# Filter products of a frequency-domain convolution as pairs of 64-row tiles, two steps at a time

## The chip, the core and the metric

The kernel runs on one core of one Trainium2 chip. The metric is the device time of one execution in microseconds (us), the median of several runs. TensorE, here PE, multiplies a stationary operand, which a weight load (PEld) puts into its array, by a moving operand that streams past it, and writes to PSUM, which has eight banks of 512 fp32 columns. VectorE is DVE, ScalarE is ACT, GpSimd is POOL, and SP is the engine whose queue issues most of the DMA transfers.

## The reference

```python
# x, v: (1, 12480, 128); pos_emb: (12480, 64); w1: (64, 64); w2: (64, 128)
h_mlp = np.maximum(pos_emb @ w1, 0.0) @ w2
h_filt = h_mlp * np.exp(-0.01 * pos)[:, None]
u = x * v
L = 2 * S
Uf = np.fft.rfft(u, n=L, axis=1)
Hf = np.fft.rfft(h_filt, n=L, axis=0)
y = np.fft.irfft(Uf * Hf[None, :, :], n=L, axis=1)[:, :S, :]
x1 = x * y
# first layer, 128 -> 2048 -> 128
r = np.maximum(x1 @ moe_w_in, 0.0)
x2 = (r * r) @ moe_w_out
# second layer, 128 -> 2048 -> 128
h = x2 @ moe2_w_in
out = (np.maximum(h, 0.0) + moe2_alpha * np.minimum(h, 0.0)) @ moe2_w_out
```

The product with w2 is linear, and so the kernel takes the transform of the 64 hidden units first and multiplies their spectra by w2 afterwards. That later product is the one that the change touches.

## The kernel before

The work has three stages. In the first, PE computes the hidden units of the filter and the short transforms of 98 points (`mlp_fill`, `stage1_chunk`), and ACT and DVE copy them from PSUM to the tensors `a_r` (hidden units) and `a_u` (u). The second stage is a loop of 49 steps (K_STEPS), two frequencies of the short transform in each. The third is the inverse short transform (`first_pass`, `sum_half`) mixed into the first tiles of the two feed-forward layers, after which the layers alone remain. Everything runs in an order written out by hand for each engine, with semaphores between the engines; no scheduler moves anything.

A step k of the second stage has these parts:

- `unit_spectra(k)` on PE: two fp32 products of 128 x 128 by 128 columns. `unit_copy(k)` on ACT copies the result to `r_hat`, which has two buffers. Its 128 rows are two halves (`HALF`) of 64 hidden units, one for each half of the sequence.
- `u_spectra(k)` on PE: two fp32 products of 256 columns, which DVE reads from PSUM.
- `filter_spectra(k)` on PE: two fp32 products of `r_hat` by `w2_sb`, 256 columns. `w2_sb` holds w2 twice, on a diagonal of two 64 x 128 blocks, with zeros elsewhere (`two_copies`). The whole result of a step fills one PSUM bank (`filter_bank`). `filter_copy(k)` on ACT copies it to `filt` three times over: once as it is, and once with the two halves of the partitions exchanged.
- `spectra_products(k)` on DVE: four instructions that multiply u's spectrum by the filter's.
- `inverse(k)` on PE: four fp32 products of 256 columns. `result_copy(k)` on ACT takes the result to `g_sb`, and SP stores it.

In round k of the loop PE runs `unit_spectra(k + 2)`, `u_spectra(k)`, `filter_spectra(k + 1)` and `inverse(k - 1)`, and ACT runs `unit_copy(k + 2)`, `filter_copy(k + 1)` and `result_copy(k - 1)`. Step 0's filter product is made in the first stage. ACT also has 12 rounds with one piece of a weight matrix to round (`round_piece`), and 7 with one large load to issue (`load_raw`, `load_gate`). SP's `load_forward` brings the table that `unit_spectra` and `u_spectra` use, into five buffers, each refilled when its `u_spectra` is done.

In the profile each fp32 product stands as two weight loads and two MATMUL rows, one for each pass over the data. At the end of the second stage `first_pass` begins each of its six halves with one bf16 product of a single row (`zeros`), built with a tile of 32 rows by 128 columns; all other products of this kernel are built with the full 128 x 128.

Of the kernel before, what the change touches and what calls it, by code (L numbers as in the profile page):

```python
# [10 lines left out]
P = 128  # L11
NB, N1, R = 2, 64, 98
K_STEPS = R // 2
# [11 lines left out]
def wait(engine, semaphore, value):  # L25

    if not isinstance(value, int) or value > 0:
        engine.wait_ge(semaphore, value)
# [412 lines left out]
def long_convolution(nc, ctx, ap, g_dram, a_u, a_r, work, gt, gt_buffers, idft98_sb, zeros, alpha_sb, x1, mem, ps):  # L441
# [12 lines left out]
    def sem(name):  # L454
        return ctx.enter_context(nc.semaphore(name))
# [3 lines left out]
    def carve(*shape):  # L459
        size = int(np.prod(shape))  # L460
        taken[0] += size
        assert taken[0] <= work.shape[1], (taken[0], work.shape)
        names = "abcd"[:len(shape)]
        sizes = dict(zip(names[1:], shape[1:]))
        return work[:, taken[0] - size:taken[0]].rearrange(f"p ({' '.join(names)}) -> p {' '.join(names)}", **sizes)

    w1_sb, window_sb, w2_sb = carve(P), carve(P)[:R], carve(2 * P)
# [14 lines left out]
    r_hat, filt = carve(2, 2, P), carve(2, 2, 4 * P)  # L482
# [9 lines left out]
    HALF = slice(0, N1), slice(N1, P)  # L492

    def unit_bank(k):
        return 6 if k == 0 else 2 + k % 2

    def filter_bank(k):
        return 7 if k == 0 else 4 + k % 2

    def two_banks(b):  # L500
        return ps[:, 2 * b:2 * b + 2, :].rearrange("p b w -> p (b w)")
# [23 lines left out]
    filt_done, filt_copied = sem("filt_done"), sem("filt_copied")  # L525
# [119 lines left out]
    def tensor_program(pe):  # L645
        def mlp_fill(i):
            wait(pe, h_windowed, i - 3)
            for n in range(8):
                if n * POS % HID == 0:
                    pe.wait_ge(pos_loaded[(8 * i + n) * POS // HID], 16)  # L650
                at = slice((8 * i + n) * R, (8 * i + n + 1) * R)
                last = nc.tensor.matmul(two_banks(i % 4)[:R, n * P:(n + 1) * P], pos_sb[:, at], w1_sb,  # L652
                                        start=True, stop=True)
            last.then_inc(mlp_done, 1)

        def stage1_chunk(n):
            kind, j = chunks[n]
            if n == 0:
                pe.wait_ge(dft98_loaded, 16)
            if n < 3:  # L660
                pe.wait_ge(h_windowed, MLP_FILLS if kind == "r" else MLP_FILLS - 3 + n)
            else:
                pe.wait_ge(copied_0, n - 2)
                pe.wait_ge(copied_1, n - 2)
            if kind == "u":
                pe.wait_ge(u_ready, j + 1)
            for c in range(CH):
                data = x_slots[:, j % X_SLOTS, c, :] if kind == "u" else h_sb[:, CH * j + c, :]
                last = nc.tensor.matmul(two_banks(n % 3)[:, 256 * c:256 * c + 2 * R], data,  # L669
                                        dft98_sb[:], start=True, stop=True)  # L670
            last.then_inc(spec_done, 1)

        def unit_spectra(k):
            pe.wait_ge(forward_loaded[k % FW], 16 * (k // FW + 1))
            wait(pe, r_hat_copied, k - 1)
            for i in range(2):
                last = nc.tensor.matmul(ps[:, unit_bank(k), P * i:P * (i + 1)], a_r_rows[:, 2 * k + i],  # L677
                                        forward[:, k % FW, i], start=True, stop=True)
            last.then_inc(r_hat_done, 1)

        def u_spectra(k):
            wait(pe, u_used, k - 1)
            for i in range(2):
                last = nc.tensor.matmul(ps[:, k % 2, 256 * i:256 * (i + 1)], forward[:, k % FW, i],  # L684
                                        a_u_rows[:, 2 * k + i], start=True, stop=True)
            last.then_inc(u_done, 1)

        def filter_spectra(k):
            pe.wait_ge(r_hat_copied, k + 1)
            wait(pe, filt_copied, k - 1)  # L690
            for i in range(2):
                last = nc.tensor.matmul(ps[:, filter_bank(k), 256 * i:256 * (i + 1)], r_hat[:, k % 2, i], w2_sb,  # L692
                                        start=True, stop=True)
            last.then_inc(filt_done, 1)

        def inverse(k):
            pe.wait_ge(y_ready, k + 1)
            pe.wait_ge(back_loaded[k % INV], 16 * (k // INV + 1))
            wait(pe, g_copied, k - 1)
            for i in range(2):  # L700
                out, at = ps[:, 6 + k % 2, 256 * i:256 * (i + 1)], slice(256 * i, 256 * (i + 1))
                for n in range(2):
                    last = nc.tensor.matmul(out, back[:, k % INV, i, n], products[:, k % 2, n, at],  # L703
                                            start=n == 0, stop=n == 1)
            last.then_inc(inv_done, 1)

        pe.wait_ge(w1_loaded, 16)
        for i in range(MLP_FILLS):
            mlp_fill(i)
        for n in range(len(chunks)):  # L710
            stage1_chunk(n)
            if n == EARLY_UNITS:
                pe.wait_ge(copied_0, units_end)
                pe.wait_ge(copied_1, units_end)
                unit_spectra(0)
            if n == EARLY_FILTER:
                pe.wait_ge(w2_loaded, 16)
                filter_spectra(0)
        pe.wait_ge(copied_0, len(chunks) - 1)
        pe.wait_ge(copied_1, len(chunks) - 1)  # L720
        unit_spectra(1)
        for k in range(K_STEPS + 1):
            if k + 2 < K_STEPS:
                unit_spectra(k + 2)
            if k == 0:
                pe.wait_ge(copied_0, len(chunks))
                pe.wait_ge(copied_1, len(chunks))
            if k < K_STEPS:
                u_spectra(k)
            if k + 1 < K_STEPS:  # L730
                filter_spectra(k + 1)
            if k == K_STEPS:
                first_pass(pe, 0)
            if k >= 1:
                inverse(k - 1)
        for h in (1, 2, 3, 5, 4):
            first_pass(pe, h)

# [64 lines left out]
    def scalar_program(act):  # L803
        def unit_copy(k):
            act.wait_ge(r_hat_done, k + 1)
            wait(act, filt_done, k - 1)
            nc.scalar.copy(r_hat[:, k % 2].rearrange("p r k -> p (r k)"), ps[:, unit_bank(k), :2 * P]
                           ).then_inc(r_hat_copied, 1)

        def filter_copy(k):  # L810
            act.wait_ge(filt_done, k + 1)
            wait(act, u_used, k - 1)
            out = ps[:, filter_bank(k), :]
            nc.scalar.copy(filt[:, k % 2, 0], out)
            for part in range(2):
                last = nc.scalar.copy(filt[HALF[part], k % 2, 1], out[HALF[1 - part]])
            last.then_inc(filt_copied, 1)

        def result_copy(k):
            act.wait_ge(inv_done, k + 1)  # L820
            wait(act, g_stored[k % 3], 16 * (k // 3))
            nc.scalar.copy(g_sb[:, k % 3].rearrange("p r w -> p (r w)"), ps[:, 6 + k % 2, :]).then_inc(g_copied, 1)
            if k >= K_STEPS - DIRECT:
                act.wait_ge(g_copied, k + 1)
                for q in range(k + 1 + DIRECT - K_STEPS):
                    move_rows(act, q, k, 1, half_1_loaded[q])

        def load_raw(k):
            act.wait_ge(u_done, 4 * (k + 1))
            act.dma_start(raw_shapes[k][1], raw_shapes[k][0]).then_inc(raw_loaded[k], 16)  # L830
# [16 lines left out]
        for n in range(len(chunks)):  # L847
            act.wait_ge(spec_done, n + 1)
            for part in range(2):
                src, dst = stage1_part(n, 0, part)  # L850
                last = nc.scalar.copy(dst, src)
# [3 lines left out]
            if n == EARLY_FILTER:  # L855
                filter_copy(0)
        unit_copy(1)
        pieces = {**{24 + n: n for n in range(4)}, **{34 + n: 4 + n for n in range(4)},
                  **{43 + n: 8 + n for n in range(4)}}
        for k in range(K_STEPS + 1):  # L860
            if k + 2 < K_STEPS:
                unit_copy(k + 2)
            if k + 1 < K_STEPS:
                filter_copy(k + 1)
            if k >= 1:
                result_copy(k - 1)
            if k in (14, 16, 18):
                load_raw((k - 14) // 2)
            if k in (20, 26, 32, 38):
                load_gate((k - 20) // 6)  # L870
            if k in pieces:
                round_piece(pieces[k])
# [204 lines left out]
```

## Time and profile before

| what | value |
|---|---|
| median of 3 runs | 1419.36 us (1418.54 to 1419.79) |
| the profiled execution, its own time | 1420.0 us |
| its span from the first to the last instruction | 1418.1 us |
| PE busy | 1405.2 us, 99% of the span |
| PE's weight loads busy | 1196.3 us, 84% |
| DVE busy | 1104.5 us, 78% |
| ACT busy | 1124.0 us, 79% |
| POOL busy | 70.2 us, 5% |
| granted TensorE clock | 1.000, which is 2.4 GHz |

Busy time is a sum over instructions; the end of a MATMUL row is modelled, so that rows which follow each other overlap, and the pace of a stream of them is read from their starts. Idle time is shown before the instruction that ended it, with what released it.

### The profile page before, as it was taken

The numbers are of one execution on the slowest core, as the hardware profiler recorded it, in microseconds if no ns is written. First come the engines' busy times: TensorE is split into PE (matmuls) and PEld (weight loads), VectorE is DVE, ScalarE is ACT, GpSimd is POOL, SyncE is SP. The second block draws the span as 40 slices with busy tenths as digits, with TensorE's granted clock in tenths as the row PEclk, the third lists the DMA queues.
The fourth block names the chain that finished last, engine by engine and source line by source line (L and its number), as shares of the span: only waits on it lengthen the run. The fifth ranks groups of instructions, "written<-read, shape, count | busy, mean of one in ns | idle before, by whom it ended". The sixth has DMA issues, their size and how long they took to land.

```text
span 1418.1 us, 19798 instructions
## 1 busy us (share of the span) xinstructions
PE 1405.2 (99%) x6810; PEld 1196.3 (84%) x6810; DVE 1104.5 (78%) x1350; ACT 1124.0 (79%) x1507; POOL 70.2 (5%) x61
## 2 busy tenths in 40 slices
PE   8999999999999999999999999999999999999997
PEld 8998888898888888888888888888888888888886
DVE  5876666556877887788788888888887888888887
ACT  3676677546877887788788888888888888888886
POOL 4510011211000000000000000000000000000000
PEclk9999999999999999999999999999999999999999
DMA  8545878542011011100000000000000000000000
GB/s 256 177 146 167 290 235 278 162 148 69 0 30 31 1 31 31 31 9 8 1 8 7 7 7 0 7 7 7 7 0 7 7 7 7 0 7 7 8 8 12
DMA packets 46900, 79.21 MB, mean 56 GB/s; under 512 B 4707, under 2 KB 26441, under 8 KB 46073
## 3 DMA queue, kind: packets, MB, share of 16 engines
q1 hardware_dynamic: 44505, 68.43, 15.6%
q10 hardware_dynamic: 2208, 9.99, 2.0%
q8 instruction: 35, 0.57, 0.2%
q14 instruction: 24, 0.20, 0.0%
q0 software_dynamic: 128, 0.02, 0.0%
HBM read 59.12 MB, written 19.23 MB: 55 GB/s over the span
## 4 chain that ended last, share of the span: by engine, by line
PE 94%; DVE 3%; ACT 1%; issue 1%; DMA 0%; ACTq 0%; DVEq 0%
PE ps L169 12%; PE ps L184 12%; PE ps L171 12%; PE ps L170 12%; PE ps L186 12%; PE ps L185 12%; PE ps L703 6%; PE ps L669 5%; PE ps L780 3%; PE ps L684 3%; PE ps L692 3%; PE ps L677 1%; PE ps L652 1%; DVE stage L371 1%; DVE g_lo L384 1%
## 5 line engine op out<-in xcount | busy, mean ns | idle before, releaser
L384 DVE TENSOR_TENSOR g_lo<-stage,g_hi 128x1024 fp32r<-128x1024 f32 (+2 forms) x199 | 238.7, 1200 | 169.1 <-ACT g_hi L289 169.0
L184 PE MATMUL ps<-g_hi,w_hi 128*128 128x512 f32 (+2 forms) x800 | 309.7, 387 | 5.9 <-DVE g_lo L384 4.7
L169 PE MATMUL ps<-x_hi,w_hi 128*128 128x512 f32 (+2 forms) x800 | 310.6, 388 | 0.1
L171 PE MATMUL ps<-x_lo,w_hi 128*128 128x512 f32 (+2 forms) x800 | 307.4, 384 | 0.0
L186 PE MATMUL ps<-g_lo,w_hi 128*128 128x512 f32 (+2 forms) x800 | 307.2, 384 | 0.0
L170 PE MATMUL ps<-x_hi,w_lo 128*128 128x512 f32 (+2 forms) x800 | 307.2, 384 | 0.0
L185 PE MATMUL ps<-g_hi,w_lo 128*128 128x512 f32 (+2 forms) x800 | 307.2, 384 | 0.0
L298 ACT ACTIVATE relu<-ps 128x1024 f32<-128x1024 f32 (+2 forms) x200 | 201.7, 1008 | 108.8 <-PE ps L171 106.0
L371 DVE SCALAR_TENSOR_TENSOR stage<-stage,alpha_sb 128x512 f32<-128x512 f32 (+2 forms) x400 | 276.5, 733 | 3.7 <-ACT stage L329 3.6
L329 ACT ACTIVATE stage<-ps,sign_sb 128x512 f32<-128x512 f32 (+2 forms) x400 | 251.2, 673 | 3.5 <-PE ps L171 2.0
L415 DVE TENSOR_TENSOR g_lo<-g,g_hi 128x1024 fp32r<-128x1024 f32 (+2 forms) x200 | 239.7, 1198 | 14.0 <-ACT g_hi L317 13.7
L289 ACT CAST g_hi<-stage 128x1024 fp32r<-128x1024 f32 (+2 forms) x199 | 204.2, 1026 | 44.6 <-DVE stage L371 33.9
L317 ACT CAST g_hi<-g 128x1024 fp32r<-128x1024 f32 (+2 forms) x200 | 205.9, 1030 | 18.9 <-DVE g L399 15.4
L184 PEld LDWEIGHTS ps<-g_hi,w_hi 128*128 128x128 f32 x800 | 150.2, 188 | 37.2 <-DVE g_lo L384 5.0
L169 PEld LDWEIGHTS ps<-x_hi,w_hi 128*128 128x128 f32 x800 | 150.3, 188 | 33.9 <-issue 4.2
L171 PEld LDWEIGHTS ps<-x_lo,w_hi 128*128 128x128 f32 x800 | 150.3, 188 | 29.8
L186 PEld LDWEIGHTS ps<-g_lo,w_hi 128*128 128x128 f32 x800 | 150.2, 188 | 29.7
L185 PEld LDWEIGHTS ps<-g_hi,w_lo 128*128 128x128 f32 x800 | 150.3, 188 | 29.3
L170 PEld LDWEIGHTS ps<-x_hi,w_lo 128*128 128x128 f32 x800 | 150.3, 188 | 28.0
L399 DVE TENSOR_TENSOR g<-relu 128x1024 f32<-128x1024 f32 (+2 forms) x125 | 149.7, 1198 | 7.0 <-ACT relu L298 4.7
L896 DVE TENSOR_TENSOR work<-ps,work 128x512 f32<-128x512 f32 x98 | 63.1, 687 | 60.4 <-PE ps L684 60.3
L703 PE MATMUL ps<-work 128*128 128x256 f32 x392 | 92.6, 379 | 0.0
(59 smaller groups left out, 1169.8 us busy)
## 6 DMA issues: line engine op xcount, KB each, us to landing
work<-dft_back SPq DMA_DIRECT2D x49, 256.0 KB, 3.1
g_dram<-work SPq DMA_DIRECT2D x49, 256.0 KB, 3.7
gt<-g_dram SPq DMA_DIRECT2D x12, 784.0 KB
gt<-x_seq SPq DMA_DIRECT2D x32, 196.0 KB
work<-v_seq SPq DMA_DIRECT2D x32, 196.0 KB
work<-dft_forward SPq DMA_DIRECT2D x49, 128.0 KB, 3.4
x<-x_gate ACTq DMA_DIRECT2D x4, 1560.0 KB, 8.0
out_t<-x SPq DMA_DIRECT2D x23, 256.0 KB, 2.0
```

The costliest lines, as they stand in the source:

```text
L169: nc.tensor.matmul(into[:, c, :t], w_hi[k][:, at], x_hi[layer][:, :t], start=True, stop=False)
L170: nc.tensor.matmul(into[:, c, :t], w_lo[k][:, at], x_hi[layer][:, :t], start=False, stop=False)
L171: last = nc.tensor.matmul(into[:, c, :t], w_hi[k][:, at], x_lo[layer][:, :t], start=False, stop=True)
L184: nc.tensor.matmul(acc[layer][:, :t], w_hi[k][:, at], hi[:, c], start=first, stop=False)
L185: nc.tensor.matmul(acc[layer][:, :t], w_lo[k][:, at], hi[:, c], start=False, stop=False)
L186: last = nc.tensor.matmul(acc[layer][:, :t], w_hi[k][:, at], lo[:, c], start=False, stop=end)
L289: nc.scalar.copy(g_hi[1][:, at, :, :t], g2[at][:, :, :t]).then_inc(g2_hi_ready, 1)
L317: nc.scalar.copy(g_hi[0][:, s // 2 % 2, :, :t], g1[:, :, :t]).then_inc(g1_hi_ready, 1)
L329: nc.scalar.activation(signed_h2[:, c, :t], h2_of(l2)[:, c, :t], ACT.Copy, scale=sign_sb[:, at:at + 1]).then_inc(signed_h2_ready, 1)
L371: nc.vector.scalar_tensor_tensor(out=g2[pair % 2][:, c, :t], in0=signed_h2[:, c, :t], scalar=alpha_sb[:, at:at + 1], in1=signed_h2[:, c, : ...
L384: nc.vector.tensor_tensor(g_lo[1][:, at, :, :t], g2[at][:, :, :t], g_hi[1][:, at, :, :t].bitcast(FP32), ALU.subtract).then_inc(g2_lo_ready, 1)
L415: nc.vector.tensor_tensor(g_lo[0][:, at, :, :t], g1[:, :, :t], g_hi[0][:, at, :, :t].bitcast(FP32), ALU.subtract).then_inc(g1_lo_ready, 1)
```

## The change

The filter product of a step is now made of four products in place of two: for each frequency i one with the first 64 rows of `r_hat` and the first block of `w2_sb`, and one with the other 64 rows and the other block, 128 columns each. Both are built with a tile of 64 rows by 128 columns, one at row 0 of the array and one at row 64, and they write to two different PSUM banks. Banks 4 and 5 are shared by an odd step and the even one after it, half of each bank for a step. PE makes the filter products of two steps in one go, in even rounds alone, behind a wait for the copies of all earlier ones; an odd step's copy on ACT waits for both. `unit_spectra` and `unit_copy` are called for step k + 3 at the end of round k instead of step k + 2 at its start.

```diff
-    def filter_bank(k):
-        return 7 if k == 0 else 4 + k % 2
+    def filter_banks(k):
+        return ps[:, 6:8, :2 * P] if k == 0 else ps[:, 4:6, 2 * P * ((k - 1) % 2):2 * P * ((k - 1) % 2 + 1)]
...
         def filter_spectra(k):
             pe.wait_ge(r_hat_copied, k + 1)
-            wait(pe, filt_copied, k - 1)
             for i in range(2):
-                last = nc.tensor.matmul(ps[:, filter_bank(k), 256 * i:256 * (i + 1)], r_hat[:, k % 2, i], w2_sb,
-                                        start=True, stop=True)
+                for blk in range(NB):
+                    last = nc.tensor.matmul(filter_banks(k)[:, blk, P * i:P * (i + 1)], r_hat[HALF[blk], k % 2, i],
+                                            w2_sb[HALF[blk], P * blk:P * (blk + 1)], start=True, stop=True,
+                                            tile_position=(N1 * blk, 0))
             last.then_inc(filt_done, 1)
...
         unit_spectra(1)
+        unit_spectra(2)
         for k in range(K_STEPS + 1):
-            if k + 2 < K_STEPS:
-                unit_spectra(k + 2)
...
             if k < K_STEPS:
                 u_spectra(k)
-            if k + 1 < K_STEPS:
+            if k % 2 == 0 and k + 2 < K_STEPS:
+                wait(pe, filt_copied, k + 1)
                 filter_spectra(k + 1)
+                filter_spectra(k + 2)
             if k == K_STEPS:
                 first_pass(pe, 0)
             if k >= 1:
                 inverse(k - 1)
+            if k + 3 < K_STEPS:
+                unit_spectra(k + 3)
...
         def filter_copy(k):
-            act.wait_ge(filt_done, k + 1)
+            act.wait_ge(filt_done, k + 1 + k % 2)
             wait(act, u_used, k - 1)
-            out = ps[:, filter_bank(k), :]
-            nc.scalar.copy(filt[:, k % 2, 0], out)
+            src = filter_banks(k).rearrange("p b (k c) -> p k b c", k=2)
+            dst = filt[:, k % 2].rearrange("p v (k b c) -> p v k b c", k=2, b=NB)
+            nc.scalar.copy(dst[:, 0], src)
             for part in range(2):
-                last = nc.scalar.copy(filt[HALF[part], k % 2, 1], out[HALF[1 - part]])
+                last = nc.scalar.copy(dst[HALF[part], 1], src[HALF[1 - part]])
             last.then_inc(filt_copied, 1)
...
         unit_copy(1)
+        unit_copy(2)
...
         for k in range(K_STEPS + 1):
-            if k + 2 < K_STEPS:
-                unit_copy(k + 2)
             if k + 1 < K_STEPS:
                 filter_copy(k + 1)
             if k >= 1:
                 result_copy(k - 1)
+            if k + 3 < K_STEPS:
+                unit_copy(k + 3)
```

On PE, in the order before, from round 4 of the second stage; L684 is `u_spectra`, L692 `filter_spectra`, L703 `inverse`, L677 `unit_spectra`:

```order
L684 MATMUL ps<-a_u,work 128x256 [waits u_used]
L684 MATMUL ps<-a_u,work 128x256
L692 MATMUL ps<-work 128x256 [waits filt_copied,r_hat_copied]
L692 MATMUL ps<-work 128x256
L703 MATMUL ps<-work 128x256 [waits g_copied,back_loaded3,y_ready]
L703 MATMUL ps<-work 128x256 x3
L677 MATMUL ps<-work,a_r 128x128 [waits r_hat_copied,forward_loaded2]
L677 MATMUL ps<-work,a_r 128x128
L684 MATMUL ps<-a_u,work 128x256 [waits u_used]
L684 MATMUL ps<-a_u,work 128x256
L692 MATMUL ps<-work 128x256 [waits filt_copied,r_hat_copied]
L692 MATMUL ps<-work 128x256
```

The same place in the changed kernel, where the same functions stand at L686, L694, L706 and L679:

```order
L686 MATMUL ps<-a_u,work 128x256 [waits u_used]
L686 MATMUL ps<-a_u,work 128x256
L694 MATMUL ps<-work 128x128 [waits r_hat_copied,filt_copied]
L694 MATMUL ps<-work 128x128 x3
L694 MATMUL ps<-work 128x128 [waits r_hat_copied]
L694 MATMUL ps<-work 128x128 x3
L706 MATMUL ps<-work 128x256 [waits g_copied,back_loaded3,y_ready]
L706 MATMUL ps<-work 128x256 x3
L679 MATMUL ps<-work,a_r 128x128 [waits r_hat_copied,forward_loaded2]
L679 MATMUL ps<-work,a_r 128x128
L686 MATMUL ps<-a_u,work 128x256 [waits u_used]
L686 MATMUL ps<-a_u,work 128x256
```

Two steps of filter products stand together, eight products of 128 columns in place of four of 256, and none follows the next `u_spectra`. `unit_spectra` for step k + 3 stands between `inverse(k - 1)` and `u_spectra(k + 1)` in both.

On ACT, before, at the first rounded piece of a weight matrix (L841); L807 is `unit_copy`, L814 and L816 `filter_copy`, L822 `result_copy`:

```order
L822 COPY work<-ps 128x512 [waits g_stored2,inv_done]
L841 CAST w_hi<-stage 128x512 [waits raw_loaded0]
L807 COPY work<-ps 128x256 [waits filt_done,r_hat_done]
L814 COPY work<-ps 128x512 [waits u_used,filt_done]
L816 COPY work<-ps 64x512 x2
```

The same place in the changed kernel, with the same functions at L829, L848, L813, L821 and L823:

```order
L829 COPY work<-ps 128x512 [waits g_stored2,inv_done]
L813 COPY work<-ps 128x256 [waits filt_done,r_hat_done]
L848 CAST w_hi<-stage 128x512 [waits raw_loaded0]
L821 COPY work<-ps 128x512 [waits u_used,filt_done]
L823 COPY work<-ps 64x512 x2
```

The copy of the hidden units' spectra has moved ahead of the rounded piece; the rest of ACT's order is as it was.

## Rows read from the trace of the kernel before

**Rows 1.** The page: busy time by engine, and the chain that ended last.
```profile
PE 1405.2 (99%) x6810; PEld 1196.3 (84%) x6810; DVE 1104.5 (78%) x1350; ACT 1124.0 (79%) x1507; POOL 70.2 (5%) x61
...
PE 94%; DVE 3%; ACT 1%; issue 1%; DMA 0%; ACTq 0%; DVEq 0%
```

**Rows 2.** The chain from 80 to 300 us, `inverse` 29 rounds apart: start, us, what.
```profile
93.11 1.73 PE ps L703 x8
...
206.22 1.73 PE ps L703 x8
```

**Rows 3.** Busy time in stretches of the second stage; the first column is the stretch.
```profile
150.00:170.00 20.00, 20.00 (x104) 17.88 (x103) 12.89 (x20) 13.54 (x28) 0.00 (x0) 1.00 0.90 304
...
230.00:250.00 20.00, 20.00 (x104) 17.88 (x103) 13.40 (x22) 14.55 (x29) 2.56 (x3) 1.00 0.80 271
```

**Rows 4.** One round on PE, timeline: start us, us, engine, line, operation, count.
```profile
153.18 0.61 PE L677 MATMUL ps<-work,a_r 128*128 128x128 f32 x4
153.62 1.03 PE L684 MATMUL ps<-a_u,work 128*128 128x256 f32 x4
154.49 1.03 PE L692 MATMUL ps<-work 128*128 128x256 f32 x4
155.35 1.89 PE L703 MATMUL ps<-work 128*128 128x256 f32 x8
157.08 0.61 PE L677 MATMUL ps<-work,a_r 128*128 128x128 f32 x4
```

**Rows 5.** Groups of instructions from 150 to 270 us: busy us, mean ns, idle before.
```profile
L896 DVE TENSOR_TENSOR work<-ps,work 128x512 f32<-128x512 f32 x62 | 39.9, 686 | 39.9 <-PE ps L684 39.9
L816 ACT COPY work<-ps 64x512 f32<-64x512 f32 x62 | 35.9, 580 | 0.7
...
L901 DVE TENSOR_TENSOR work<-work 128x512 f32<-128x512 f32 x31 | 21.5, 693 | 1.1
L898 DVE TENSOR_TENSOR work<-ps,work 128x512 f32<-128x512 f32 x31 | 21.1, 681 | 0.0
...
L814 ACT COPY work<-ps 128x512 f32<-128x512 f32 x31 | 18.2, 587 | 32.4 <-PE ps L692 32.4
L822 ACT COPY work<-ps 128x512 f32<-128x512 f32 x31 | 18.2, 587 | 0.8
...
L807 ACT COPY work<-ps 128x256 f32<-128x256 f32 x31 | 11.7, 377 | 0.4 <-issue 0.4
L841 ACT CAST w_hi<-stage 128x512 fp32r<-128x512 f32 x11 | 6.8, 622 | 0.0
```

**Rows 6.** Products of 98 rows and 128 columns in a row, timeline, PE.
```profile
286.38 3.74 PE L747 MATMUL ps<-idft_sb,gt 98*128 98x128 f32 x32
...
291.57 1.95 PE L747 MATMUL ps<-idft_sb,stage 98*128 98x128 f32 x16
```

**Rows 7.** The one-row products in a 32-row tile and their neighbours, timeline, PE.
```profile
276.01 0.38 PE L703 MATMUL ps<-work 128*128 128x256 f32 x1
276.32 0.39 PE L762 MATMUL ps<-rest_of_a_r 1*128 1x512 bf16 x1
276.63 1.16 PE L747 MATMUL ps<-idft_sb,gt 98*128 98x128 f32 x8
...
280.86 0.39 PE L762 MATMUL ps<-rest_of_a_r 1*128 1x512 bf16 x1
...
282.26 0.39 PE L762 MATMUL ps<-rest_of_a_r 1*128 1x512 bf16 x1
```

**Rows 8.** The weight loads at the same place, timeline, PEld.
```profile
276.31 0.09 PEld L762 LDWEIGHTS ps<-rest_of_a_r 1*128 1x128 bf16 x1 [0.33 <-issue]
276.63 0.41 PEld L747 LDWEIGHTS ps<-idft_sb,gt 98*128 98x128 f32 x3 [0.23 <-issue]
```

**Rows 9.** `unit_copy` on ACT after the last of rows 4, timeline.
```profile
157.83 0.38 ACT L807 COPY work<-ps 128x256 f32<-128x256 f32 x1
```

**Rows 10.** The 49 transfers of `load_forward` (L584), its source line's view.
```profile
DMA to landing us min/median/max: 1.9/3.4/9.4
```

## The prediction

> **What bounds the kernel now.** I read the page first: PE is busy for 99% of the span and makes up 94% of the chain that ended last [rows 1]. An edit that shortens PE's stream therefore shortens the time, as long as no other engine takes its place. The chain through the second stage then gives the pace of a round: 29 rounds lie between the two rows of `inverse`, (206.22 - 93.11) / 29 = 3.900 us [rows 2]. The table of stretches says that nothing else is near this: in 20 us PE is busy for 20.00, ACT for 13.5 to 14.6, DVE for 12.9 to 13.4, and the clock stands at 1.00 [rows 3]. The timeline of one round on PE takes it apart by starts, since ends are modelled [rows 4]: `u_spectra` 0.87 us, `filter_spectra` 0.86, `inverse` 1.73, `unit_spectra` 0.44, together 3.90 with no gap. A pass of 256 columns so costs 1.73 / 8 = 0.216 us. The groups of the stage show the same from the other side: DVE's first instruction and ACT's `filter_copy` wait for PE 39.9 and 32.4 us in 31 rounds, 1.3 and 1.0 us in each, and no row of PE waits for them [rows 5].
>
> **What the change removes.** Rounds 0, 2, ..., 46 have filter products, 24 groups for 48 steps. Two steps cost PE 2 x 4 passes x 0.216 = 1.73 us now.
>
> **What it adds, the passes.** Two steps become eight fp32 products of 128 columns, 16 passes, each with its own weight load. What a pass of 128 columns costs is read where many stand in a row: (3.74 - 1.95) / 16 = 0.112 us [rows 6]; the four of `unit_spectra` take 0.44, 0.11 each [rows 4]. One after another the 16 would take 1.79 us, a little more than now. All of the gain thus hangs on whether a tile at row 0 and one at row 64 work at the same time, their weight loads as well. No row of before shows two tiles beside each other, so I bound it from both sides: 16 slots of 0.112 us if they don't, 8 if they share perfectly. The order written in the code lies between. Each fp32 product issues its two passes back to back on one tile, and only then comes the other tile. If products start in order, a product's first pass can run beside its predecessor's second pass and no earlier; each further product then adds one slot, and eight take 9 slots, 9 x 0.112 = 1.01 us. I take this one.
>
> **What it adds, the switches.** The array must go from 128 rows to 64-row tiles and back, once for each group. The trace has a near case: the six one-row products that are built with a 32-row tile [rows 7]. From one to the next is 282.26 - 280.86 = 1.40 us. In it are 8 passes of 0.112 = 0.90 and the one-row pass of 512 columns, whose row lasts 0.39 us like that of a pass of 256 fp32 columns at 0.38, so 0.216. The rest, 0.29 us, is the price of the excursion. It splits up: the last pass of `inverse` ends at 276.01 + 0.216 = 276.23 and the next starts at 276.32, 0.09 later; that one ends at 276.54 and the next starts at 276.63, again 0.09. The remaining 0.11 is a weight load that isn't hidden: the loads start at 276.31 and 276.63 with their products, not ahead of them [rows 8], and the eight passes behind it last 1.16 us, where 7 x 0.112 + 0.275 (the modelled length of one, 3.74 less 31 x 0.112) is 1.06. The one-row product's own load was cheap, a filter product's is one of 128 fp32 columns, so I add another 0.11: 0.40 us for an excursion. Its bounds are 0 (if 64-row tiles need no switch) and 0.40.
>
> At this place two rules of the Trainium skill part. "TensorE: Matmul & The Clock Gate", LDWEIGHTS, says that a weight load takes its columns divided by 1.2, whatever the rows, which makes 107 ns for 128 columns; by this, with loads one at a time, a group's 16 loads would be 1.71 us as an estimate, nothing would be won, and the kernel would take some 1429 us. "TensorEngine Tiling (Array Packing)", Key Properties, says that different tiles can load and multiply in parallel, and by its twofold speedup the time would be some 1409 us as an estimate. No row of before decides between them.
>
> **The sum.** A group costs 1.01 + 0.40 = 1.41 us instead of 1.73, saving 0.32; 24 groups save 7.7 us. Step 0's filter product, in the first stage, has an excursion for itself: 5 slots, 0.56, plus 0.40 is 0.96 instead of 0.86, a loss of 0.1. Net 7.6 us. The profiled execution took 1420.0 us and would take 1412.4; it lies 0.6 above the median of the runs, 1419.4, and so the median becomes **1411.8 us**.
>
> **What I cost at nothing.** `unit_spectra(k + 3)` is moved in the text alone: on PE it stands in the same place. ACT's rounded piece now stands behind `unit_copy`, not ahead of it, which only helps PE. The new waits, then. PE's second filter product of a group needs `unit_copy(k + 2)`, made just before `u_spectra(k)`: a `unit_copy` ends 157.83 + 0.38 - 157.08 = 1.13 us after `unit_spectra` starts [rows 4, 9], and is needed at 0.44 + 0.87 + 0.2 (switch and load) + half of 1.01, which is 2.0. The harder case is a whole group's ACT work. I count from the end of a group and allow 0.2 us from a last pass to its copy (the row of four passes lasts 1.03, their pace makes 0.87 [rows 4]): the copies of the odd step 0.2 to 2.0 (0.59 + 2 x 0.58 [rows 5]); `inverse(k - 1)` ends at 0.2 + 1.73 = 1.9, its copy at 2.7, `unit_copy` at 3.1, a piece (0.62) at 3.7, the even step's copies at 5.5; `inverse(k)` ends at 1.9 + 0.44 + 0.87 + 1.73 = 5.0, its copy at 6.1, `unit_copy(k + 4)` at 6.5. PE needs this last for the second step of the next group at 5.0 + 0.44 + 0.87 + 0.2 + 0.5 = 7.0. A margin of 0.5 us is left even with a piece, so ACT (5.5 us in 7.5, 6.7 with two pieces) should hide. DVE's 2.7 us for a step (2 x 0.686 + 0.681 + 0.693 [rows 5]) lie between `u_spectra(k)` and `inverse(k)`; that distance on PE is at least 1.73 + 0.44 + 0.87 = 3.0 without the group, plus a group of 1.4, since exactly one stands in it: 4.4. If ACT's cover were gone, each 0.1 us by which it is late would cost 2.4 us over 24 groups. Behind the waiting product on PE stands `inverse`, and behind that everything.
>
> The forward table has less time: from the end of `u_spectra(k)` to `unit_spectra(k + 5)` were 3 x 3.90 - 0.44 - 0.87 = 10.4 us; where only one group lies between (odd k) it becomes 10.4 - 3 x 0.86 + 1.41 = 9.2. The slowest load landed after 9.4 us, the median after 3.4 [rows 10]. One late load may cost some 0.3 us. The third stage begins without a gap on PE other than the excursions above [rows 7], and the loads it waits for are issued by step, so they move with it; I expect the gain of the second stage at the end.
>
> **The rivals.**
> - **The tiles work one at a time** (slower). Mechanism: the weight loads of both tiles pass one after another at 0.112 us. For it speaks that loads and passes of 128 columns already run at the same 0.11 pace; against it only that the two tiles use different rows. A group costs 16 x 0.112 + 0.40 = 2.19, 0.46 more than now; 24 of them 11.0, and 0.4 for step 0 (8 x 0.112 + 0.40 = 1.30): about **1431 us**. The point from which it decides is (1.73 - 0.40) / 0.112 = 11.9 slots for a group.
> - **Partial overlap**, 11 to 13 slots, because a tile's loads don't run beside the other's passes as freely: a group gains 0.10 or loses 0.13, 1417 to 1423 us; about the same at 12.
> - **No switch to pay**: 64-row tiles don't drain, or the loads are prefetched across the switch. A group is then 0.9 to 1.1 us, saving 0.6 to 0.8, so 1400 to 1405 us. The excursions [rows 7] speak against it.
> - **ACT is late**: the second step of a group waits 0.3 us for `unit_copy`, by the margin above a miss of 0.8. The gain is gone: about 1419 us.
>
> **How the numbers follow.** The forecast (8 to 10 slots, an excursion of 0.29 to 0.40) has 0.62 and the range 1406 to 1415. One tile at a time has 0.19, partial overlap 0.11, no switch 0.05, ACT late 0.03. A measurement of this kernel tells no change from one of about 0.2%, 2.8 us. Faster: 0.62 + 0.05 + 0.03 of the partial case = 0.70; same: 0.05 + 0.03 = 0.08; slower: 0.19 + 0.03 = 0.22. A range of 1403 to 1425 leaves out one tile at a time, and part of the case without a switch.
>
> **What would show it.** Right: the starts of two `inverse` groups around a filter group and those without one tell the group's cost directly, 1.4 us; the round's pace alternates between 3.04 and 4.45 us; the first weight load of a group starts 0.09 us after the last pass ends, and the products of the two tiles start in pairs. Wrong: filter passes that follow each other every 0.112 us throughout (one at a time), an idle row on PE before the filter products released by `unit_copy` (ACT late), or one before `unit_spectra` released by a load.

## The result, and the profile after

| | before | changed |
|---|---|---|
| median of the runs | 1419.51 us (4 runs, 1418.54 to 1419.79) | 1409.63 us (4 runs, 1409.35 to 1411.36) |
| the profiled execution's own time | 1420.0 us | 1411.36 us |
| its span | 1418.1 us | 1409.6 us |
| PE busy | 1405.2 us | 1394.9 us |
| ACT, DVE busy | 1124.0, 1104.5 us | 1121.8, 1104.4 us |

The ratio is 0.9934, with an interval of 0.9923 to 0.9946: the change makes the kernel 9.9 us faster by the medians. The profiled execution is the slowest of the four and only 8.6 us faster than the profiled one of before; where the difference went stands below.

The page of the changed kernel has the same shape as [rows 1], but DMA makes up 2% of the chain that ended last, where it was 0%; the forward tables are 1% of it.

```profile
PE 1394.9 (99%) x7006; PEld 1179.8 (84%) x7006; DVE 1104.4 (78%) x1350; ACT 1121.8 (80%) x1507; POOL 69.5 (5%) x61
...
PE 93%; DVE 3%; DMA 2%; ACT 1%; issue 1%; ACTq 0%; DVEq 0%
```

The timeline of PE over two rounds of the changed kernel, to be held against [rows 4]; L694 is now `filter_spectra`, L706 `inverse`, L679 `unit_spectra`, L686 `u_spectra`:

```profile
153.04 1.03 PE L686 MATMUL ps<-a_u,work 128*128 128x256 f32 x4
154.00 1.16 PE L694 MATMUL ps<-work 64*128 64x128 f32 x16
155.09 1.99 PE L706 MATMUL ps<-work 128*128 128x256 f32 x8
156.92 0.61 PE L679 MATMUL ps<-work,a_r 128*128 128x128 f32 x4
157.37 1.03 PE L686 MATMUL ps<-a_u,work 128*128 128x256 f32 x4
158.23 1.89 PE L706 MATMUL ps<-work 128*128 128x256 f32 x8
159.96 0.61 PE L679 MATMUL ps<-work,a_r 128*128 128x128 f32 x4
160.40 1.03 PE L686 MATMUL ps<-a_u,work 128*128 128x256 f32 x4
```

A round with a group lasts 157.37 - 153.04 = 4.33 us, one without 160.40 - 157.37 = 3.03 us, so the group costs 1.29 to 1.30, against 1.73 for the two of before. It takes apart as the prediction did, except for one term. `u_spectra` ends at 153.04 + 0.87 = 153.91 and the group starts at 154.00, 0.09 later. The row of 16 passes lasts 1.16 us, exactly as long as the row of 8 passes behind a one-row product in [rows 7]: the passes of the two tiles fill 8 slots, not 9. Behind the group the first row of `inverse` starts at 155.09, and the eight passes last 1.99 instead of 1.89: one weight load that isn't hidden.

The weight loads show the two tiles side by side. This is PEld at the same place, the second row a narrower stretch of the same stream:

```profile
154.00 0.97 PEld L694 LDWEIGHTS ps<-work 64*128 64x128 f32 x16 [0.33 <-issue]
...
154.00 0.19 PEld L694 LDWEIGHTS ps<-work 64*128 64x128 f32 x2 [0.33 <-issue]
```

Two loads begin at 154.00 and together last 0.19 us, the length of one; two more begin every 0.11 us after them. Whatever one load costs, the second beside it is free.

Where the profiled execution lost time is in its waits. The view of waits from 80 to 285 us (waiting engine and line, released by, us in total, times, longest) has three that stand on PE in the second stage and are not there before: the 25 changes into the 64-row tiles, 0.33 us each as weight loads see them, two late tables, and two waits of `inverse` for DVE. The timeline, in the second fence, shows the longer wait for a table:

```profile
PEld ps L694 <- issue: 8.2, 25, 0.3
PEld ps L679 <- DMA work<-dft_forward: 2.4, 2, 1.6
PEld ps L706 <- DVE work L909: 1.0, 2, 0.5
```

```profile
172.96 1.89 PE L706 MATMUL ps<-work 128*128 128x256 f32 x8
176.02 0.71 PE L679 MATMUL ps<-work,a_r 128*128 128x128 f32 x4 [1.17 <-DMA work<-dft_forward]
```

`inverse` ends its stream at 172.96 + 1.73 = 174.69 and `unit_spectra` starts 1.33 us later, since its table is not there; it was issued at 165.79 and took 10.18 us to land, as the chain that ended last says:

```profile
165.79 10.18 DMA work<-dft_forward
```

From its issue to the moment when PE was ready are 174.69 - 165.79 = 8.9 us, the room that five buffers leave here. The second late table made PE wait 0.60 us. Before, no instruction on PE waited for a table.

The two waits for DVE stand at the two ends of the loop. The first is that of the first `inverse`:

```profile
90.73 1.03 PE L686 MATMUL ps<-a_u,work 128*128 128x256 f32 x4
91.87 2.00 PE L706 MATMUL ps<-work 128*128 128x256 f32 x8
```

`u_spectra` ends its stream at 90.73 + 0.87 = 91.60, `inverse` starts 0.27 us later, and its first weight load isn't hidden (2.00 against 1.89). The last `inverse` of the loop loses the same: `u_spectra` starts at 264.73, `inverse` at 265.88. Together they cost some 0.7 us.

### The profile page after: what moved, and what is told of

It is laid out like the page before. It is cut to its first block, busy times and chain, and to the rows that moved or that the text cites. A ratio compares the mean times of both kernels' runs of the same rounds, so it can differ in the third digit from the quotient of the medians.

```text
span 1409.6 us, 20167 instructions
## 1 busy us (share of the span) xinstructions
PE 1394.9 (99%) x7006; PEld 1179.8 (84%) x7006; DVE 1104.4 (78%) x1350; ACT 1121.8 (80%) x1507; POOL 69.5 (5%) x61
## 4 chain that ended last, share of the span: by engine, by line
PE 93%; DVE 3%; DMA 2%; ACT 1%; issue 1%; ACTq 0%; DVEq 0%
PE ps L169 12%; PE ps L184 12%; PE ps L171 12%; PE ps L170 12%; PE ps L186 12%; PE ps L185 12%; PE ps L706 5%; PE ps L671 5%; PE ps L786 3%; PE ps L686 3%; PE ps L694 2%; DMA work<-dft_forward 1%; PE ps L679 1%; PE ps L654 1%; DVE stage L371 1%; DVE g_lo L384 1%
## 5 line engine op out<-in xcount | busy, mean ns | idle before, releaser
L706 PE MATMUL ps<-work 128*128 128x256 f32 x392 | 95.2, 386 | 0.2
```

## The experiments

Times are medians; the kernel before had a median of 1419.37 to 1419.88 in the four jobs. "The changed kernel" is at 1409.63 in the result above and at 1409.72 in one of these jobs.

**One step's products in every round.**

```diff
-            if k % 2 == 0 and k + 2 < K_STEPS:
-                wait(pe, filt_copied, k + 1)
-                filter_spectra(k + 1)
-                filter_spectra(k + 2)
+            if k + 1 < K_STEPS:
+                wait(pe, filt_copied, k + 1)
+                filter_spectra(k + 1)
...
-            act.wait_ge(filt_done, k + 1 + k % 2)
+            act.wait_ge(filt_done, k + 1)
```

> The changed kernel, but PE makes one step's filter products in every round, so that there are 48 excursions into the 64-row tiles in place of 24. Theory A (an excursion costs a fixed 0.40 us, 0.09 us at each side and a weight load of 0.11 us that isn't hidden at each side): a group of four products costs 4 x 0.112 + 0.40 = 0.85 us, each round is 3.04 + 0.85 = 3.89 us, and the time is 24 x 0.40 = 9.6 us above the changed kernel's, about 1419. Theory B (the price is small, and the gain comes from something else in the new order): rounds of some 3.5 us and a time near 1410 or less.

Measured: 1418.92 us (1418.22 to 1419.53), ratio to the kernel before 0.9997 (0.9987 to 1.0006). Its timeline on PE:

```profile
152.45 1.03 PE L686 MATMUL ps<-a_u,work 128*128 128x256 f32 x4
153.41 0.71 PE L694 MATMUL ps<-work 64*128 64x128 f32 x8
154.05 1.99 PE L706 MATMUL ps<-work 128*128 128x256 f32 x8
155.88 0.61 PE L679 MATMUL ps<-work,a_r 128*128 128x128 f32 x4
156.33 1.03 PE L686 MATMUL ps<-a_u,work 128*128 128x256 f32 x4
```

A round is 3.88 us, and 3.03 of it are the other products: a single step in tiles costs 0.85, where the full array takes 0.86. Theory A holds. With one step at a time the tiles win nothing at all; the price of the excursion is as large as the gain.

**The new order on the full array.**

```diff
-        return ps[:, 6:8, :2 * P] if k == 0 else ps[:, 4:6, 2 * P * ((k - 1) % 2):2 * P * ((k - 1) % 2 + 1)]
+        return ps[:, 7, :] if k == 0 else ps[:, 4 + (k - 1) % 2, :]
...
-                for blk in range(NB):
-                    last = nc.tensor.matmul(filter_banks(k)[:, blk, P * i:P * (i + 1)], r_hat[HALF[blk], k % 2, i],
-                                            w2_sb[HALF[blk], P * blk:P * (blk + 1)], start=True, stop=True,
-                                            tile_position=(N1 * blk, 0))
+                last = nc.tensor.matmul(filter_banks(k)[:, 256 * i:256 * (i + 1)], r_hat[:, k % 2, i], w2_sb,
+                                        start=True, stop=True)
...
-            src = filter_banks(k).rearrange("p b (k c) -> p k b c", k=2)
-            dst = filt[:, k % 2].rearrange("p v (k b c) -> p v k b c", k=2, b=NB)
+            src = filter_banks(k)
+            dst = filt[:, k % 2]
```

> The new order (two steps of filter products in even rounds, hidden units three steps ahead, the new waits), but the products as before on the full 128 x 128 array, 256 columns each, one bank a step. Theory A (the gain is all in the tiles): a group costs 1.73 us, two rounds 7.80, the time is that of before, 1419.5 within 0.5. Theory B (the order itself gives something or costs something, by waits of ACT or DVE): clearly below 1418 or above 1421.

Measured: 1419.79 us (1418.96 to 1420.89), ratio 1.0002 (0.9993 to 1.0012). The new order, its waits and the moved `unit_copy` are worth nothing and cost nothing that the medians show; the whole gain is in the tiles. From the first to the last pass of `u_spectra` it takes 185.3 us, as before.

**The tiles in turn.**

```diff
-            for i in range(2):
-                for blk in range(NB):
+            for blk in range(NB):
+                for i in range(2):
```

> The changed kernel, but in a step both products of the tile at row 0 come first and then both of the tile at row 64. Theory A (PE takes products in order, and two that follow each other on different tiles share their slots): a group is 5 times two slots, not 4 times, so 0.22 us longer, and the time some 5 us above the changed kernel's, about 1415. Theory B (each tile has a stream of its own that runs ahead freely): no difference, 1409.6. My slots of the prediction (a product starts with the second pass of the one before it): seven or more slots a step.

Measured: 1412.26 us (1411.76 to 1412.63), 2.6 above the changed kernel; between the two theories, and both fall as they were put. So does the third of the expectations, with seven or more slots a step. The rows, the last three from stretches of the weight loads that end ever later:

```profile
155.11 1.26 PE L694 MATMUL ps<-work 64*128 64x128 f32 x16
...
155.11 0.20 PEld L694 LDWEIGHTS ps<-work 64*128 64x128 f32 x2 [0.33 <-issue]
...
155.11 0.53 PEld L694 LDWEIGHTS ps<-work 64*128 64x128 f32 x8 [0.33 <-issue]
...
155.11 0.63 PEld L694 LDWEIGHTS ps<-work 64*128 64x128 f32 x9 [0.33 <-issue]
```

The group is one slot longer, 1.26 against 1.16, and 24 x 0.10 = 2.4 us. Yet two loads begin within 0.02 us of each other at 155.11, where on one tile they begin 0.11 us apart, and although here the second tile's first product stands behind both products of the first tile. So the tiles do run ahead of each other, past at least one product of the other tile, but not without limit. The trace shows where the slot goes: the first step's eight loads begin in pairs, in four slots; the ninth, the first of the second step, begins alone, then come three pairs, and the last is alone again. In the second step the two tiles thus run one slot apart. Why they do so there, and not in the first step, stays open.

**All products on one tile.** (The second block's products read the first 64 rows of both operands, so half of the filter spectra is not computed.)

```diff
-                    last = nc.tensor.matmul(filter_banks(k)[:, blk, P * i:P * (i + 1)], r_hat[HALF[blk], k % 2, i],
-                                            w2_sb[HALF[blk], P * blk:P * (blk + 1)], start=True, stop=True,
-                                            tile_position=(N1 * blk, 0))
+                    last = nc.tensor.matmul(filter_banks(k)[:, blk, P * i:P * (i + 1)], r_hat[HALF[0], k % 2, i],
+                                            w2_sb[HALF[0], P * blk:P * (blk + 1)], start=True, stop=True,
+                                            tile_position=(0, 0))
```

> The changed kernel, but all eight products of a group on the tile at row 0 (the second block's products read the first 64 rows of both operands, so that half of the filter spectra is wrong). This prices the rival of one tile at a time: 16 slots of 0.112 us and 0.40 us for the excursion, 2.19 us a group in place of 1.29, 24 x 0.9 = 21.5 us above the changed kernel's, about 1431. If the two tiles only seemed to run together, the time would be that of the changed kernel, 1409.6.

Measured: 1430.52 us (1430.23 to 1431.28), ratio 1.0079 (1.0063 to 1.0096).

```profile
153.65 2.05 PE L694 MATMUL ps<-work 64*128 64x128 f32 x16
155.63 1.99 PE L706 MATMUL ps<-work 128*128 128x256 f32 x8
```

The row of 16 passes is 2.05 us long, 0.89 more than in the changed kernel: eight slots of 0.111. This is the slower rival of the prediction, priced there at 1431. The instructions are the same in number and kind and write to the same banks; what decides is the place in the array, with the rows of the operands that belong to it.

**Half of the work on one tile.** (From step 3 on, the products of the tile at row 64 are left out.)

```diff
+                    if blk == 0 or k < 3:
```

> The changed kernel without the products of the tile at row 64 (from step 3 on; half of the filter spectra is left out). Theory A (the second tile is free, loads and all): 8 slots a group as in the changed kernel, the same time, 1409.6 within 0.5. Theory B (part of the second tile's work is paid for, by loads or by the issue of instructions): a faster kernel; each 10 ns of a slot would show as 24 x 0.08 = 1.9 us.

Measured: 1411.38 us (1409.28 to 1413.57). The median says neither A nor B; the profile does:

```profile
153.56 1.03 PE L686 MATMUL ps<-a_u,work 128*128 128x256 f32 x4
154.52 1.16 PE L695 MATMUL ps<-work 64*128 64x128 f32 x8
...
157.88 1.03 PE L686 MATMUL ps<-a_u,work 128*128 128x256 f32 x4
```

Eight passes last 1.16 us, the sixteen of the changed kernel as well, and the round is 4.32 against 4.33. The second tile is free to within 10 ns a group. The profiled execution, at 1410.97, explains its own time without a cost of the products: PE waits three times for a forward table, 1.7 us in all. Of the slowest one, 1413.57, there is no trace, and why it took so long is not shown.

**Six buffers for the forward tables.**

```diff
-    FW, INV = 5, 4
+    FW, INV = 6, 4
```

> The changed kernel with six buffers for the forward tables in place of five, so that a load may take one more step. Theory A (the two waits for a table in the changed kernel's profile, 2.1 us in all, are due to loads of 10.2 and 9.5 us that have only 9.0 us of room where one group of filter products lies between): no such wait is left, the profiled execution takes about 1409.3, the median falls by 0 to 1 us. Theory B (the loads are late because the DMA engines are full, and a deeper buffer only moves the wait to another table or store): the sum of PE's waits for DMA stays at 1 us or more.

Measured: 1409.11 us (1408.74 to 1409.96), ratio 0.9929 (0.9916 to 0.9943). No wait of PE for a table is left. But the slowest load of this execution landed after 9.0 us, hardly more than the 8.9 that five buffers leave, so this profile alone proves little:

```profile
DMA to landing us min/median/max: 2.0/3.6/9.0
```

**Four buffers for the forward tables.**

```diff
-    FW, INV = 5, 4
+    FW, INV = 4, 4
```

> The changed kernel with four buffers for the forward tables in place of five. By PE's order the room for a load, from the end of the u_spectra that frees the buffer to the unit_spectra that needs it, is then 1.73 + 0.44 + 0.87 + 1.29 + 1.73 = 6.1 us in every round, where five buffers leave 9.1 or 10.4 us and six leave 13.4. Theory A (PE waits for a table exactly where a load lands later than its room): about one load in six took 6.1 us or more in the earlier profiles, by 0.2 to 4 us, so PE waits for a table some 5 to 10 times, 5 to 12 us in all, and the time is 1415 to 1421 us. Theory B (the late loads are shifted or caused by something that the number of buffers does not touch): still two or three waits and 2 to 3 us, about 1410.

Measured: 1422.71 us (1420.39 to 1426.58), ratio 1.0022 (1.0012 to 1.0032), slower than the kernel before. The waits of its profiled execution:

```profile
PEld ps L679 <- DMA work<-dft_forward: 12.6, 9, 3.1
ACT work L813 <- PE ps L679: 10.3, 6, 2.8
```

Nine waits and 12.6 us, with loads no slower than elsewhere (median 3.1 us, slowest 8.7). Theory A had the mechanism and five to ten waits, and put the time 2 us too low. What decides is how much room PE's order and the number of buffers leave a load. Taking that room from 6.1 to 9.1 us, by PE's rows, is worth 13 us.

**The change again, for its spread.** (No edit.)

> The changed kernel as it is, for the spread of its times beside the other two. Theory A (its waits for late forward tables come and go from one execution to the next): a median near 1409.8 with single times up to 1411.5 or more, against a spread of about 1.2 us with six buffers. Theory B (the profiled execution was an exception): all times within 0.6 us of 1409.5.

Measured: 1409.72 us (1408.79 to 1412.04). The profiled execution, at 1412.04, has a load of 11.7 us, and PE waits three times for a table:

```profile
  PEld ps L679: 2.3, 3
...
DMA to landing us min/median/max: 2.0/3.5/11.7
```

The late loads come and go between executions, as theory A has it. Their place does not. These are the changed kernel's loads in the first profile, those issued from 70 to 142 us and those from 142 to 178 us, and the large load that ACT issues just ahead of the slowest one:

```profile
DMA to landing us min/median/max: 2.0/3.0/4.1
...
DMA to landing us min/median/max: 3.4/6.6/10.2
```

```profile
164.94 0.36 ACTq L842 DMA_DIRECT2D x<-x_gate  x1
```

ACT issues seven large loads, at 142.85, 150.27, 157.57, 164.94, 188.46, 210.55 and 233.34 us; the two late tables, at 165.79 and 211.40, come 0.85 us behind two of them. In every one of the thirteen profiles, before and after, each table that took more than 5.3 us was issued within 9.5 us behind one of these seven. The large load of 1 to 1.5 MB beside a table is thus the likely cause of its being late; it is not shown, since no run moves the large loads.

**The rounded piece first.**

```diff
-            if k + 3 < K_STEPS:
-                unit_copy(k + 3)
             if k in (14, 16, 18):
                 load_raw((k - 14) // 2)
...
             if k in pieces:
                 round_piece(pieces[k])
+            if k + 3 < K_STEPS:
+                unit_copy(k + 3)
```

> The changed kernel, but ACT rounds its piece of a weight matrix and issues its large loads before it copies the hidden units' spectra, as before the change. Theory A (ACT has about 0.5 us to spare even with a piece in each round): the same time, 1409.6 within 0.5. Theory B (the margin was only there because the copy moved ahead): PE waits for unit_copy ahead of the second step's filter products in the even rounds with a piece, up to 0.1 us in 6 of them, or more where I mis-sized ACT's chain, and the time rises by 1 us or more.

Measured: 1410.20 us (1409.40 to 1411.00). No row of PE waits for `unit_copy`; two wait for a table, 1.2 us as weight loads see it. The difference of 0.6 us to the changed kernel lies within the spread that these waits make. ACT's margin is there without the move.

**128 rows of zeros.** The price of an excursion was read off the six one-row products [rows 7]; this takes their small tile away.

```diff
-        zeros = sb("rest_of_a_r", [P, 2 * (R * 2 * HID - 6 * F)], mybir.dt.bfloat16)[:1]
+        zeros = sb("rest_of_a_r", [P, 2 * (R * 2 * HID - 6 * F)], mybir.dt.bfloat16)[:P]
```

> The changed kernel, but the six products of zeros that begin the inverse transform's halves have 128 rows of zeros and the full array in place of one row and a 32-row tile. Theory A (the 0.29 us that I read off their places is the price of changing the tile size, and of nothing else such as the change of data type): from one to the next 1.11 us in place of 1.40, 6 x 0.29 = 1.7 us less in all, the median about 1.7 us below that of the changed kernel in this job. Theory B (the price belongs to the bf16 product as such): the same 1.40 us, and no gain.

Measured: 1408.44 us (1408.24 to 1409.81), 1.3 below the changed kernel in the same job.

```profile
270.62 0.38 PE L768 MATMUL ps<-rest_of_a_r 128*128 128x512 bf16 x1
270.84 1.05 PE L753 MATMUL ps<-idft_sb,gt 98*128 98x128 f32 x8
271.73 0.38 PE L768 MATMUL ps<-rest_of_a_r 128*128 128x512 bf16 x1
```

From one to the next it is 271.73 - 270.62 = 1.11 us, not 1.40, and the bf16 product itself fills 0.22. The 0.29 us was thus no price of the bf16 product as such. The edit changes the number of rows together with the tile, but a change from 98 to 128 rows alone, both on the full array, costs nothing in the same trace: 267.79 - 266.89 = 0.90 us are eight passes.

```profile
266.89 1.06 PE L753 MATMUL ps<-idft_sb,gt 98*128 98x128 f32 x8
267.79 1.89 PE L706 MATMUL ps<-work 128*128 128x256 f32 x8
```

By the trace the six are worth 1.7 us; the medians give 1.3, with a spread as wide as the difference.

**Both together.**

```diff
-    FW, INV = 5, 4
+    FW, INV = 6, 4
...
-        zeros = sb("rest_of_a_r", [P, 2 * (R * 2 * HID - 6 * F)], mybir.dt.bfloat16)[:1]
+        zeros = sb("rest_of_a_r", [P, 2 * (R * 2 * HID - 6 * F)], mybir.dt.bfloat16)[:P]
```

> Both together on the changed kernel: six buffers for the forward tables and 128 rows of zeros. If the two effects add, no wait of PE for a table, 1.11 us from one product of zeros to the next, and a median of about 1409.1 - 1.7 = 1407.4.

Measured: **1407.77 us** (1407.21 to 1408.60), ratio 0.9918 (0.9904 to 0.9931), the fastest version here and 1.95 us below the changed kernel in the same job. In its profiled execution a load issued in an odd round took 9.2 us, more than the 8.9 that five buffers leave there, and PE waited for none.

## Why the prediction was right, point by point

- **The bound.** PE's stream set the time, and what was taken out of it came back as time. From the first to the last pass of `u_spectra` the stage takes 274.3 - 89.0 = 185.3 us before, 265.4 - 88.1 = 177.3 after, and 263.2 - 88.0 = 175.2 where no table is late, with six buffers; the version with 128 rows of zeros, in whose profile no table was late either, has 264.4 - 89.2 = 175.2 as well. 24 x (1.73 - 1.29) is 10.6, and the measured 10.1 is nearly this less the wait for DVE at the start of the stage.
- **The passes, 9 slots.** Mis-sized: 8. I argued that a product's first pass can run beside the second pass of its predecessor and no earlier, and thus lost one slot a group. In the trace both tiles start together, and the experiment with the tiles in turn shows that PE reaches past a whole product for work on the other tile. The slot of 0.112 us is right: 8 x 0.111 on one tile. The one term is 24 x 0.11 = 2.7 us.
- **The excursion, 0.40 us.** Right, term by term: 0.09 us ahead of the group, one load of 0.11 in the row of 1.16, and 0.09 and 0.11 behind. That it was read off a 32-row tile and held for a 64-row tile, the experiments with one step in each round (0.85 us for 4 slots) and with 128 rows of zeros confirm. The rule of the Trainium skill that I left out of the sum belongs here: "TensorEngine Tiling (Array Packing)", Key Properties, says that a change of tiling mode drains the engine. The trace agrees: 0.09 us without a pass at each side.
- **The weight loads.** The two pages of the Trainium skill that the prediction names did not contradict each other after all. "TensorE: Matmul & The Clock Gate", LDWEIGHTS, in the Trainium skill, has a load's time right for one tile: 107 ns by its formula, and in the traces a load that nothing hides makes a row 0.10 to 0.11 us longer, with 64 rows (1.16 against 1.05 us) as with 128 (1.99 against 1.89). "TensorEngine Tiling (Array Packing)", Key Properties, in the Trainium skill, is right that another tile's load runs beside it: 16 loads begin in 8 slots. The error would have been to apply the first across tiles.
- **What was costed at nothing.** For ACT, the new waits and the new order this is confirmed by the pairs on the full array (1419.79) and by the rounded piece first. For DVE it holds inside the loop, but not at its ends. The prediction's shortest way on PE from `u_spectra(k)` to `inverse(k)`, 1.73 + 0.44 + 0.87 = 3.0 us plus a group, does not exist there: for the first `inverse` there is no earlier one to run and the way is 1.29 + 0.44 + 0.87 = 2.6, for the last there is no group and no `unit_spectra`, and it is 1.73 + 0.87 = 2.6, against the 2.7 us that DVE needs. These are the two waits of the section on the result, some 0.7 us. Before, another filter product stood in both places and PE did not wait.
- **The forward tables.** The place was right for both late tables of the first profile (an odd step, with one group between, 9.1 us of room by the rows and 8.9 in the trace); in the profile of the change run again the slowest load belonged to an even step, with a group more. The size was not: I named 0.3 us beside the sum, and the profiled executions of the changed kernel lost about 2 us of PE's time in two or three waits, because the slowest load took 10.2 and 11.7 us instead of 9.4. One execution of before was too few to bound the slowest of 49 loads: the table issued right behind the first load of `x_gate` took 6.5 us there, and 7.1 to 10.2 in the twelve other profiles. In the medians it is less, perhaps half a microsecond: the version with six tables is 0.5 to 0.7 us faster in both comparisons, which their spread does not settle.
- **The sum.** Forecast 1411.8, measured 1409.63, 2.2 us lower. The slot gives 2.7 and another 0.1 in step 0's product; against it stand the two waits for DVE, 0.7, and the late tables, 0.5 in the medians. That leaves 1.6 of the 2.2. The other 0.6 is not taken apart; it lies within what executions differ by ahead of the second stage, whose first `u_spectra` starts at 87.7 to 89.2 us in the thirteen profiles. That the forecast came so near is thus in part luck: a term too dear by 2.8 us met two that were not in the sum.

## What to carry to other kernels

A product whose stationary operand is block diagonal can be cut into tiles that run beside each other, weight loads included; the second tile is free, but in this kernel each change of tile size on PE cost 0.09 us plus a weight load that nothing hid, and so such products must be gathered until the gain outweighs two changes. Look for small tiles elsewhere, too: a one-row product in a stream of full ones cost 0.29 us more than one with 128 rows. Check the first and the last round of a loop by themselves, since a margin that holds inside can be missing there. And when a stream gets faster or its work is regrouped, count the room of every prefetch anew in the round with the least between release and use, and hold it against the slowest transfer of several executions, not against the median of one; look as well which large transfer it runs beside.

## What the runs showed of the hardware

- The loads and passes of a tile at row 0 and one at row 64 start within 0.01 us of each other and keep the pace of one tile, 0.111 us a pass of 128 fp32 columns.
- With the tiles in turn, a product for the other tile starts 0.02 us behind the first one, past a whole product (two loads, two passes) that stands ahead of it and whose loads begin 0.22 us later; one slot a group is still lost, in the second step.
- The row of a pass of 512 bf16 columns is as long with 1 row (0.38 to 0.39 us) as with 128 (0.38); what the one-row product costs beyond it, 0.29 us, is gone with its 32-row tile.
- Tables of 128 KB land after 1.9 to 5.3 us, and after up to 11.7 us when they are issued within 9.5 us behind a load of 1 to 1.5 MB.
